# Moving the split of two weights from the recurrence's loop into its last tiles and the routing

## The chip, the cores and the metric

The program runs on one core of a Trainium2 chip, as one launch. The metric is the device time of one execution in microseconds (us), as the median of several runs. The kernel before takes 721.05 us (three runs, 720.83 to 721.4). For a change of this size a difference under about 0.2% (1.4 us) can't be told from none.

## The reference

Three stages follow one another, on 3072 tokens of width 384:

```python
# 1: gated linear recurrence; B, H, S, D = 4, 8, 768, 48
f = 1.0 / (1.0 + np.exp(-f_logit))
for t in range(S):
    state = f[:, :, t, :, None] * state + np.einsum('bhd,bhe->bhde', k[:, :, t], v[:, :, t])
    y[:, :, t] = np.einsum('bhd,bhde->bhe', q[:, :, t], state)
...
# 2: routing of each token to one of E = 8 experts by cosine, two layers (384 -> 1024 -> 384)
expert_idx = np.argmax(logits, axis=1)
h = np.maximum(x[mask] @ w1[e], 0.0)
out[mask] = gate_w[mask, None] * (h @ w2[e])
...
# 3: the gated block
a = x @ w1
b = x @ w2
h = a * b @ w3
return (h @ w_out).astype(np.float32)
```

Since nothing stands between the last two products, the kernel multiplies the weights first: `w34 = w3 @ w_out`, of 1024 x 384. It must be exact to nearly fp32, so every large product is made of three fp32r products: each operand is split into a high half (a rounded copy) and a low half (the whole less the high half), and hi\*hi + hi\*lo + lo\*hi is summed. This case is about where the high and low halves of `w3` and `w_out` are made.

## The kernel before, in words

**Recurrence.** 24 tiles of 128 time steps (NT = 24) are worked through in steps s = -3 to 24. Each engine has its own program, and `steps` gives all of them the same frame: steps -3 to 4 written out, steps 5 to 20 as a hardware loop of four steps a turn (m, u), steps 21 to 24 written out. In one step several tiles are in flight at different stages; `tile_of(s, lag)` says which tile a part of the step works on. The order in a step is fixed by hand on each engine, and the engines meet by semaphores alone:

- TensorE (PE): `scores` (L691) of tile s, `cumulate` (L682, L683) of s+2, `rows_and_logits` (L744) of s-1, `turn_qk` (L735) of s+1, then `state_products` (L703), `chunk_products` (L724) and `update_products` (L714) of s.
- ScalarE (ACT): `copy_yT` (L995) of s-1, the logarithms (L966 to L971) of s+3, the exponentials (L979, L981) of s+2, `copy_qT` (L986) of s+1, `square` (L998) of s-1. `rows_and_logits` of a tile waits for its `copy_yT`.
- VectorE (DVE): `carry` (L1212), `scale_k` (L1189), `mask` (L1205), `bound` (L1195), `take_rows` (L1224, L1226), `copy_kT` (L1200), `low_logs` (L1179). `scores` of the next tile waits for `copy_kT`.
- GpSimd (POOL): `decay` (L566), `clamp` (L552), `scale_q` (L558).

**The weights' halves in the loop.** SyncE loads one row block of `w3` (transposed, 128 x 1024) and one of `w_out` (128 x 384) every two steps. In each loop step ScalarE makes the high half of half a row block of `w3` (`high_w3`, L1010, 512 elements a partition) at the step's start and of half a block of `w_out` (`high_wo`, L1004, 192) at its end; GpSimd makes the low half of `w3` (`low_w3`, L575) and VectorE that of `w_out` (`low_wo`, L1174). In the profile numbers and endings are left out of names: `w_hi<-w_sb` at L1010 is `w3_hi`, `w_lo<-w_sb,w_hi` at L575 is `w3_lo`, and `w<-b_a` at L1081 is `w34_hi`.

**The end of the recurrence and the routing.** In step 23 VectorE looks for the smallest decay (`find_least`, L1270), and in step 24 TensorE turns that column (L793) and VectorE makes a flag of it. Then VectorE alone runs the routing: a chain of small instructions, each waiting for the one before (`link`), from L1357 to L1463. TensorE fills this time with the eight products of `w34` (`w34_product(f1)`, 24 matmuls each, L765 to L767) and takes part in the chain at four places, in this order: products 0 and 1, the ranks (L833, L834, wait for `rank_in`, set by the scan at L1365), products 2 and 3, the first list (L839, waits for `list_in`, set by L1390), products 4 and 5, the full list (L846), `turn(0)` (L857, waits for the first four gathers of GpSimd, L624, which wait for the `ids` made of the first list), products 6 and 7. Then come the experts' slots, from 182.47 us on, and the gated block.

**SBUF.** The halves of both weights lie over tiles of later stages; `w3_hi` overwrites `w3_sb` from one row block behind.

Of the kernel before, what the change touches and what calls it, by code (L numbers as in the profile page):

```python
# [27 lines left out]
P = 128  # L28
# [23 lines left out]
TURN_AT = 3  # L52
LISTS = 5
# [9 lines left out]
RING = 4  # L63
# [49 lines left out]
def build(nc, ctx, qkvf, emb, tau, sets1, sets2, w3_t, w_out, out):  # L113
# [22 lines left out]
    w3_lo = low_w3.enter_context(nc.sbuf_tensor("w3_lo", [P, KF, KF, P], F32R))  # L136
# [11 lines left out]
    early("rest_of_w3_lo", [P, KF * FF - KF * 2 * DM])  # L148
    x_all = early("x_all", [P, (RING + 1) * DM])
    wo_lo = early("wo_lo", [P, KF, DM], F32R)  # L150
    above = ExitStack()
    w3_hi = above.enter_context(nc.sbuf_tensor("w3_hi", [P, KF, FF], F32R))
    above.close()
    early("first_w3_hi", [P, FF])
    w3_sb = early("w3_sb", [P, KF, FF])
# [3 lines left out]
    early("first_wo_hi", [P, DM])  # L159
    wo_sb = early("wo_sb", [P, KF, DM])  # L160
    early("up_to_rows", [P, 1216])
# [141 lines left out]
    w3_hi_done, w3_lo_done, wo_lo_done = sem("w3_hi_done"), sem("w3_lo_done"), sem("wo_lo_done")  # L303
# [224 lines left out]
    def _(pool):  # L528
# [40 lines left out]
        def low_w3(m, u):  # L569

            rows = bass.ds(m * 2 - 2 + u // 2, 1)
            cols, places = slice(u % 2 * FF // 2, (u % 2 + 1) * FF // 2), slice(u % 2 * KF // 2, (u % 2 + 1) * KF // 2)
            by_place = lambda ap: ap.rearrange("p a (f n) -> p f (a n)", n=P)
            pool.wait_ge(w3_hi_done, m * 8 + (2 * u - 7))
            pool.tensor_tensor(w3_lo[:, places, rows, :].rearrange("p f a n -> p f (a n)"),  # L575
                               by_place(w3_sb[:, rows, cols]), by_place(w3_hi[:, rows, cols].bitcast(F32)),
                               ALU.subtract).then_inc(w3_lo_done, 1)
# [41 lines left out]
        pool.sem_inc(w3_lo_done, 2)  # L619
# [8 lines left out]

        pool.wait_ge(x_done, NT)
# [40 lines left out]
    def _(pe):  # L670
# [98 lines left out]
        def w34_product(f1, blocks=range(KF)):  # L769
            if 0 in blocks:  # L770
                pe.wait_ge(w3_lo_done, 2 * KF + 2)
                pe.wait_ge(wo_lo_done, 2 * KF + 2)
                if f1 >= 4:
                    pe.wait_ge(w34_hi_done, f1 - 3)
                    pe.wait_ge(w34_lo_done, f1 - 3)
            for f2 in blocks:
                cols = slice(f1 * P, (f1 + 1) * P)
                mm = three(W34_BANKS[f1 % 4][:, 0:DM], w3_hi[:, f2, cols], w3_lo[:, f1, f2, :], wo_hi[:, f2, :],
                           wo_lo[:, f2, :], f2 == 0, f2 == KF - 1)
            if KF - 1 in blocks:  # L780
                mm.then_inc(w34_done, 1)
# [181 lines left out]
    def _(act):  # L963
# [36 lines left out]
        def high_wo(m, u):  # L1000
            rows, half = bass.ds(m * 2 - 2 + u // 2, 1), slice(u % 2 * DM // 2, (u % 2 + 1) * DM // 2)
            act.wait_ge(w3_in[u // 2], m * 32)
            act.wait_ge(wo_lo_done, m * 4 + (u - 3))
            act.copy(wo_hi[:, rows, half], wo_sb[:, rows, half]).then_inc(w3_hi_done, 1)  # L1004

        def high_w3(m, u):
            rows, half = bass.ds(m * 2 - 2 + u // 2, 1), slice(u % 2 * FF // 2, (u % 2 + 1) * FF // 2)
            act.wait_ge(w3_in[u // 2], m * 32)
            act.wait_ge(w3_lo_done, m * 4 + (u - 3))
            act.copy(w3_hi[:, rows, half], w3_sb[:, rows, half]).then_inc(w3_hi_done, 1)  # L1010

        def step(s, r, part=None):
            if part:
                high_w3(*part)
# [17 lines left out]
            if part:  # L1032
                high_wo(*part)
# [6 lines left out]

        act.wait_ge(flag_done, 1)
# [121 lines left out]
    def _(dve):  # L1163
# [68 lines left out]
        def low_wo(m, u):  # L1232

            rows, half = bass.ds(m * 2 - 2 + u // 2, 1), slice(u % 2 * DM // 2, (u % 2 + 1) * DM // 2)
            dve.wait_ge(w3_hi_done, m * 8 + (2 * u - 6))
            low(wo_lo[:, rows, half], wo_sb[:, rows, half], wo_hi[:, rows, half]).then_inc(wo_lo_done, 1)

        def step(s, r, part=None):
# [74 lines left out]
        dve.sem_inc(wo_lo_done, 2)  # L1313
# [288 lines left out]
```

## Time and profile before

| | |
|---|---|
| median of 3 runs | 721.05 us |
| the profiled execution | 719.52 us, of which the span (first to last instruction) is 717.6 us |
| TensorE busy | 704.7 us, 98% of the span, granted clock 0.999 |
| VectorE, ScalarE, GpSimd busy | 347.1, 292.1, 193.8 us |
| loop steps 5 to 20 | 38.17 to 124.46 us (starts of `scores` of tiles 5 and 20) |
| steps 21 to 24 | 129.89 to 145.9 us |
| routing with the products of `w34` | 145.9 to 182.5 us |
| experts and gated block | 182.5 to 717.6 us |

The span is read as a row of stages in which TensorE is nearly always busy. What an edit is worth is then how much TensorE's idle time in its stage grows or shrinks. The instructions' times count from the start of the span.

### The profile page before, as it was taken

To read this page: it belongs to the slowest core of one execution; us is meant where nothing else is said; L and a number is where in the kernel's file an instruction comes from. 1 tells how busy PE (TensorE), PEld (TensorE's weight loads), DVE (VectorE), ACT (ScalarE), POOL (GpSimd) and SP (SyncE) were. 2 spreads that over 40 slices of the span, in tenths; PEclk is the share of its full clock that TensorE was granted. 3 is DMA by queue.
4 is the path that set the end of the run, shared out by engine and by line. 5 is a ranking of instruction groups with operands and counts; after the bars stand their busy time and mean duration, and the time that the engine had idled before them with its cause. 6 is when DMAs were issued, how large, how long until landed. Compare 5 with 4: busy or idle time off the path is not lost.

```text
span 717.6 us, 13946 instructions
## 1 busy us (share of the span) xinstructions
PE 704.7 (98%) x4863; PEld 642.2 (89%) x4863; DVE 347.1 (48%) x564; ACT 292.1 (41%) x559; POOL 193.8 (27%) x197
## 2 busy tenths in 40 slices
PE   7999999999999999999999999999999999999997
PEld 6988988899999999999999988988988989889887
DVE  6899999768764545546465431212212112112121
ACT  6777888525353435535445342123022022121220
POOL 4567777202322021100000003024033051150242
PEclk9999999999999999999999999999999999999999
DMA  7788886261745443434243330000000010000001
GB/s 221 225 242 227 235 237 176 67 186 58 222 146 161 132 132 99 139 114 133 89 119 118 112 90 1 1 22 23 0 33 11 0 44 0 11 33 0 22 22 44
DMA packets 73056, 70.79 MB, mean 99 GB/s; under 512 B 20520, under 2 KB 61480, under 8 KB 73024
## 3 DMA queue, kind: packets, MB, share of 16 engines
q1 hardware_dynamic: 69952, 60.95, 29.2%
q0 software_dynamic: 3072, 9.44, 4.1%
q8 instruction: 17, 0.28, 0.2%
q14 instruction: 15, 0.12, 0.1%
HBM read 60.88 MB, written 9.49 MB: 98 GB/s over the span
## 4 chain that ended last, share of the span: by engine, by line
PE 79%; DVE 2%; issue 1%; ACT 1%; POOL 1%; DMA 0%; POOLq 0%; ACTq 0%; DVEq 0%
PE b_a L765 10%; PE b_a L767 10%; PE b_a L766 10%; PE bank L767 9%; PE bank L765 9%; PE bank L766 9%; PE b_y L765 6%; PE b_y L766 6%; PE b_y L767 6%; PE bank L857 1%; PE bank L744 1%; PE b_y L724 1%; PE bank L735 1%; PE b_a L691 1%; DMA xs<-x_recurrence,ids 0%
## 5 line engine op out<-in xcount | busy, mean ns | idle before, releaser
L650 POOL TENSOR_TENSOR p_lo<-prod,p_hi 128x512 fp32r<-128x512 f32 x42 | 54.0, 1285 | 333.2 <-ACT p_hi L1149 333.2
L1146 ACT COPY a_sb<-b_a 128x512 f32<-128x512 f32 x48 | 28.3, 589 | 218.2 <-PE bank L767 218.2
L1551 DVE TENSOR_TENSOR prod<-bank,a_sb 128x512 f32<-128x512 f32 x48 | 33.2, 692 | 165.7 <-ACT a_sb L1146 165.7
L1507 DVE SCALAR_TENSOR_TENSOR h_lo<-b_a,h_hi 128x432 fp32r<-128x432 f32 x64 | 38.9, 607 | 96.0 <-ACT h_hi L1099 94.4
L1099 ACT ACTIVATE h_hi<-b_a 128x432 fp32r<-128x432 f32 x64 | 34.1, 532 | 124.2 <-PE b_a L767 116.3
L1174 DVE TENSOR_TENSOR w_lo<-w_raw,w_hi 128x768 fp32r<-128x768 f32 x72 | 67.9, 956 | 5.4 <-ACT w_hi L1062 1.2
L766 PE MATMUL b_a<-x_lo,w_hi 128*128 128x432 f32 x192 | 68.7, 358 | 0.0
L767 PE MATMUL b_a<-x_hi,w_lo 128*128 128x432 f32 x192 | 68.7, 358 | 0.0
L765 PE MATMUL b_a<-x_hi,w_hi 128*128 128x432 f32 x192 | 68.7, 358 | 0.0
L1062 ACT CAST w_hi<-w_raw 128x768 fp32r<-128x768 f32 x72 | 58.5, 834 | 0.0
L765 PE MATMUL b_a<-m_hi,w_hi 128*128 128x512 f32 x144 | 56.1, 390 | 0.7 <-DVE w_lo L1174 0.7
L767 PE MATMUL b_a<-m_hi,w_lo 128*128 128x512 f32 x144 | 56.1, 390 | 0.0
L766 PE MATMUL b_a<-m_lo,w_hi 128*128 128x512 f32 x144 | 56.1, 390 | 0.0
L765 PE MATMUL bank<-m_hi,w_hi 128*128 128x512 f32 x144 | 56.0, 389 | 0.0
L766 PE MATMUL bank<-m_lo,w_hi 128*128 128x512 f32 x144 | 56.0, 389 | 0.0
L767 PE MATMUL bank<-m_hi,w_lo 128*128 128x512 f32 x144 | 56.0, 389 | 0.0
L624 POOL DMA_INDIRECT xs<-x_recurrence,ids x24 | 26.0, 1084 | 110.9 <-PE bank L857 76.3
L765 PE MATMUL b_y<-h_hi,w_hi 128*128 128x432 f32 x128 | 46.9, 366 | 0.2
L766 PE MATMUL b_y<-h_lo,w_hi 128*128 128x432 f32 x128 | 45.8, 358 | 0.0
L767 PE MATMUL b_y<-h_hi,w_lo 128*128 128x432 f32 x128 | 45.8, 357 | 0.0
L766 PEld LDWEIGHTS b_a<-x_lo,w_hi 128*128 128x128 f32 x192 | 36.2, 188 | 1.4
L765 PEld LDWEIGHTS b_a<-x_hi,w_hi 128*128 128x128 f32 x192 | 36.1, 188 | 1.5
(247 smaller groups left out, 1630.2 us busy)
## 6 DMA issues: line engine op xcount, KB each, us to landing
w_raw<-sets SPq DMA_DIRECT2D x80, 192.0 KB, 3.8
w_raw<-sets SPq DMA_DIRECT2D x40, 384.0 KB, 4.6
ring_all<-qkvf SPq DMA_DIRECT2D x24, 384.0 KB, 3.9
ring_fc<-qkvf SPq DMA_DIRECT2D x24, 192.0 KB, 3.8
ring_all<-qkvf SPq DMA_DIRECT2D x24, 192.0 KB, 2.7
x_recurrence<-x_all SPq DMA_DIRECT2D x24, 192.0 KB, 3.5
w_sb<-w_t SPq DMA_DIRECT2D x8, 512.0 KB, 4.7
wo_sb<-w_out SPq DMA_DIRECT2D x8, 192.0 KB, 3.8
```

Source lines behind the costliest of these rows:

```text
L624: pool.indirect_dma_start(out=xs[:, w % BATCH, :], out_offset=None, in_=rec_dram.rearrange("b c p n -> (b c p) n"), in_offset=bass.Indirec ...
L650: pool.tensor_tensor(p_lo[:, f, :], prod[:, f % 2, :], p_hi[:, f, :].bitcast(F32), ALU.subtract).then_inc(pl_done, 1)
L691: mm = pe.matmul([b_a0, b_a1][g][:, j * P:(j + 1) * P], kT[g * HP:(g + 1) * HP, r % 2, j, :], qT[g * HP:(g + 1) * HP, r % 2, j, :], start= ...
L765: pe.matmul(acc, a_hi, b_hi, start=first, stop=False, skip_group_check=skip)
L766: pe.matmul(acc, a_hi, b_lo, start=False, stop=False, skip_group_check=skip)
L767: return pe.matmul(acc, a_lo, b_hi, start=False, stop=last, skip_group_check=skip)
L1062: act.copy(piece(w_hi, f), piece(w_raw, f)).then_inc(wh_done, 1)
L1099: act.activation(h_hi[:, f % 2, 0:SW], b_h[f % 2][:, 0:SW], ACT.Relu).then_inc(hh_done, 1)
L1146: act.copy(a_sb[:, f % 2, :], b_a[f % 2][:]).then_inc(as_done, 1)
L1174: return dve.tensor_tensor(out_, whole, high.bitcast(F32), ALU.subtract)
L1507: dve.scalar_tensor_tensor(out=h_lo[:, f % 2, 0:SW], in0=b_h[f % 2][:, 0:SW], scalar=0.0, in1=h_hi[:, f % 2, 0:SW].bitcast(F32), op0=ALU.m ...
L1551: dve.tensor_tensor(prod[:, f % 2, :], b_b[f % 2][:], a_sb[:, f % 2, :], ALU.mult).then_inc(pr_done, 1)
```

## The change

Nothing of the two weights is split in the loop any more; both are still loaded there. The work is done whole-block by whole-block:

- ScalarE makes the high half of `w_out` in two casts of 1536 elements a partition (steps 21 and 23) and that of `w3` in eight casts of 1024 (a column block f1 each): block 0 in step 21, 1 in step 22, 2 in step 23, 3 behind step 24, 4 and 5 behind the square root of the norms, 6 and 7 behind the first two copies of `w34`.
- VectorE makes the low half of `w_out` in two instructions of 1536 elements, at the end of steps 22 and 23.
- GpSimd makes the low half of `w3`, two instructions of 512 elements a block: block 0 in step 22, block 1 in step 23, blocks 2 to 7 behind the steps and ahead of the first gathers.
- TensorE waits for each product's own block, not for all of them.
- `low_logs` stands right behind `bound` on VectorE, ahead of `take_rows` and `copy_kT`.
- The raw, high and low blocks of `w3` share one tile and partly overwrite each other, three blocks apart; the SBUF layout follows.

```diff
-        def low_w3(m, u):
-            rows = bass.ds(m * 2 - 2 + u // 2, 1)
...
-            pool.wait_ge(w3_hi_done, m * 8 + (2 * u - 7))
-            pool.tensor_tensor(w3_lo[:, places, rows, :].rearrange("p f a n -> p f (a n)"),
...
+        def low_w3(f1):
+            pool.wait_ge(w3_hi_done, f1 + 1)
+            if f1 >= LOW_HEAD:
+                pool.wait_ge(w3_lo_done, f1 * 2)
+            for part in (slice(0, KF // 2), slice(KF // 2, KF)):
+                pool.tensor_tensor(w3_lo(f1)[:, part], w3_raw(f1)[:, part], w3_hi(f1)[:, part].bitcast(F32), ALU.subtract
+                                   ).then_inc(w3_lo_done, 1)
...
-            if part:
-                low_w3(*part)
+            if isinstance(s, int) and s == NT - 2:
+                low_w3(0)
             if isinstance(s, int) and s == NT - 1:
                 whole_constants()
                 counted_constants()
+                low_w3(1)
...
+        for f1 in range(2, KF):
+            low_w3(f1)
         pool.wait_ge(x_done, NT)
...
-                pe.wait_ge(w3_lo_done, 2 * KF + 2)
-                pe.wait_ge(wo_lo_done, 2 * KF + 2)
+                pe.wait_ge(w3_lo_done, f1 * 2 + 2)
+                pe.wait_ge(wo_lo_done, 1)
...
+            if KF - 1 in blocks:
+                pe.wait_ge(wo_lo_done, 2)
...
+        def high_wo(half):
+            rows = slice(half * KF // 2, (half + 1) * KF // 2)
+            act.wait_ge(w3_in[1], 16 * KF)
+            need(act, wo_lo_done, half)
+            act.copy(wo_hi[:, rows, :], wo_sb[:, rows, :]).then_inc(wo_hi_done, 1)
+
+        def high_w3(f1):
...
+            need(act, w3_lo_done, (f1 - HIGH_AHEAD + 1) * 2)
+            act.copy(w3_hi(f1), w3_raw(f1)).then_inc(w3_hi_done, 1)
 
         def step(s, r, part=None):
-            if part:
-                high_w3(*part)
             if (i := tile_of(s, -1)) is not None:
                 copy_yT(i)
...
-            if part:
-                high_wo(*part)
+            if isinstance(s, int) and s == NT - 3:
+                high_wo(0)
+                high_w3(0)
+            if isinstance(s, int) and s == NT - 2:
+                high_w3(1)
+            if isinstance(s, int) and s == NT - 1:
+                high_wo(1)
+                high_w3(2)
...
+        high_w3(3)
         act.wait_ge(flag_done, 1)
...
+        high_w3(4)
+        high_w3(5)
         for f1 in range(KF):
             act.wait_ge(w34_done, f1 + 1)
             act.copy(w34_hi[:, f1, :], W34_BANKS[f1 % 4][:, 0:DM]).then_inc(w34_hi_done, 1)
+            if f1 < 2:
+                high_w3(6 + f1)
...
+        def low_wo(half):
+            rows = slice(half * KF // 2, (half + 1) * KF // 2)
+            dve.wait_ge(wo_hi_done, half + 1)
+            low(wo_lo[:, rows, :], wo_sb[:, rows, :], wo_hi[:, rows, :]).then_inc(wo_lo_done, 1)
...
             if (i := tile_of(s, 2)) is not None:
                 bound(i)
+            if (i := tile_of(s, 3, 1)) is not None:
+                low_logs(i, r + 3)
...
-            if (i := tile_of(s, 3, 1)) is not None:
-                low_logs(i, r + 3)
-            if part:
-                low_wo(*part)
+            if isinstance(s, int) and s in (NT - 2, NT - 1):
+                low_wo(s - (NT - 2))
             if isinstance(s, int) and s == NT - 1:
                 find_least()
                 scale_experts()
```

The order of instructions at two places shows what moves. First ScalarE from the last `square` of the loop's tiles to the routing, before (`yT` is `copy_yT`, `x_all,nsq` is `square`):

```order
L998 ACTIVATE x_all,nsq<-x_all 128x384 [waits nsq_done,x_done]
L995 COPY yT<-b_y 128x512 [waits xl_at,y_done]
L986 COPY qT<-bank 128x512 [waits sp_done,tr_done]
L1027 ACT_TABLE_LOAD
L1027 ACTIVATE rt<-nsq 128x8 [waits rl_done]
L998 ACTIVATE x_all,nsq<-x_all 128x384 [waits nsq_done,x_done]
L995 COPY yT<-b_y 128x512 [waits xl_at,y_done]
L998 ACTIVATE x_all,nsq<-x_all 128x384 [waits nsq_done,x_done]
L995 COPY yT<-b_y 128x512 [waits xl_at,y_done]
```

And the same stretch of ScalarE in the changed kernel, whose line numbers are other (`w_high<-w_all` is a block of `w3`), up to the last copy of `yT`, which follows it:

```order
L1006 ACTIVATE x_all,nsq<-x_all 128x384 [waits nsq_done,x_done]
L1012 CAST wo_hi<-wo_sb 128x1536 [waits w3_in1]
L1018 CAST w_high<-w_all 128x8x128 [waits w3_in1,w3_in0]
L1003 COPY yT<-b_y 128x512 [waits xl_at,y_done]
L994 COPY qT<-bank 128x512 [waits sp_done,tr_done]
L1033 ACT_TABLE_LOAD
L1033 ACTIVATE rt<-nsq 128x8 [waits rl_done]
L1006 ACTIVATE x_all,nsq<-x_all 128x384 [waits nsq_done,x_done]
L1018 CAST w_high<-w_all 128x8x128 [waits w3_in1,w3_in0]
L1003 COPY yT<-b_y 128x512 [waits xl_at,y_done]
L1006 ACTIVATE x_all,nsq<-x_all 128x384 [waits nsq_done,x_done]
L1012 CAST wo_hi<-wo_sb 128x1536 [waits wo_lo_done,w3_in1]
```

Each of the three copies of `yT` now stands behind one or two casts. Second, GpSimd behind the steps, before (constants of the routing, then the first gather):

```order
L587 IOTA steps_k 128x56
L589 IOTA slot_no 1x152
L591 IOTA lane_no 128x1
L592 IOTA tile_no 128x24
L594 IOTA win_no 128x24
L595 IOTA row_no 128x128
L624 DMA xs<-x_recurrence,ids 128x384 [waits x_stored2,x_stored3,x_stored1,ids_done,x_stored0,x_done]
```

And in the changed kernel from the second instruction of block 2 on:

```order
L581 TENSOR_TENSOR w_lo_head<-w_all,w_high 128x512 [waits w3_hi_done]
L581 TENSOR_TENSOR w_lo_head<-w_all,w_high 128x512
L581 TENSOR_TENSOR w_lo_head<-w_all,w_high 128x512 [waits w3_hi_done]
L581 TENSOR_TENSOR w_lo_head<-w_all,w_high 128x512
L581 TENSOR_TENSOR w_lo_head<-w_all,w_high 128x512 [waits w3_hi_done]
L581 TENSOR_TENSOR w_lo_head<-w_all,w_high 128x512
L581 TENSOR_TENSOR w_high<-w_all,w_high 128x4x128 [waits w3_lo_done,w3_hi_done]
L581 TENSOR_TENSOR w_high<-w_all,w_high 128x4x128
L581 TENSOR_TENSOR w_high<-w_all,w_high 128x4x128 [waits w3_lo_done,w3_hi_done]
L581 TENSOR_TENSOR w_high<-w_all,w_high 128x4x128
L629 DMA xs<-x_recurrence,ids 128x384 [waits x_stored2,x_stored3,x_stored1,ids_done,x_stored0,x_done]
```

Ten of these instructions belong to blocks 3 to 7; GpSimd had nothing to do there before.

## Rows read from the trace of the kernel before

**Rows 1.** The page: busy time, share of the span and instructions of each engine.
```profile
PE 704.7 (98%) x4863; PEld 642.2 (89%) x4863; DVE 347.1 (48%) x564; ACT 292.1 (41%) x559; POOL 193.8 (27%) x197
```
**Rows 2.** The timeline of TensorE: start us, us, engine line op, out<-in.
```profile
16.25 1.16 PE L691 MATMUL b_a<-qT,kT 64*128 64x128 f32 x16
...
21.68 1.16 PE L691 MATMUL b_a<-qT,kT 64*128 64x128 f32 x16
...
101.83 1.16 PE L691 MATMUL b_a<-qT,kT 64*128 64x128 f32 x16
...
129.89 1.16 PE L691 MATMUL b_a<-qT,kT 64*128 64x128 f32 x16
```
**Rows 3.** The timeline of VectorE and GpSimd in two loop steps.
```profile
102.22 0.55 DVE L1189 TENSOR_TENSOR ks<-ring_all,en 128x384 f32<-128x384 f32 x1
102.29 1.62 POOL L575 TENSOR_TENSOR w_lo<-w_sb,w_hi  x1 [1.24 <-ACT w_hi L1010]
...
107.74 1.28 POOL L575 TENSOR_TENSOR w_lo<-w_sb,w_hi  x1 [1.20 <-ACT w_hi L1010]
107.85 1.59 DVE L1189 TENSOR_TENSOR ks<-ring_all,en 128x384 f32<-128x384 f32 x1
...
108.99 0.82 POOL L566 TENSOR_TENSOR state<-s_sum,e_all 128x192 f32<-128x192 f32 x1
```
**Rows 4.** The timeline of VectorE, one loop step.
```profile
99.89 0.69 DVE L1200 COPY kT<-bank 128x512 f32<-128x512 f32 x1
```
**Rows 5.** Groups by line and shape: count, busy us, mean ns, idle before.
```profile
L966 ACT ACTIVATE ef<-ring_fc 128x384 f32<-128x384 f32 x24 | 12.6, 525 | 2.3 <-DVE ring_fc L1296 2.3
L1010 ACT CAST w_hi<-w_sb x16 | 9.9, 617 | 0.0
```
**Rows 6.** The page's groups of instructions, same columns.
```profile
L1146 ACT COPY a_sb<-b_a 128x512 f32<-128x512 f32 x48 | 28.3, 589 | 218.2 <-PE bank L767 218.2
...
L1062 ACT CAST w_hi<-w_raw 128x768 fp32r<-128x768 f32 x72 | 58.5, 834 | 0.0
```
**Rows 7.** Instructions by their line: ns min/median/max, first and last start, forms.
```profile
L650 POOL TENSOR_TENSOR p_lo<-prod,p_hi x42: 1279/1285/1297, 427.0 to 698.2; 128x512 fp32r<-128x512 f32 x42
...
L1174 DVE TENSOR_TENSOR m_lo<-mT,m_hi x8: 1758/1759/1760, 336.8 to 651.2; 128x1536 fp32r<-128x1536 f32 x8
```
**Rows 8.** The timeline of ScalarE, last tiles.
```profile
134.56 0.19 ACT L998 ACTIVATION_READ_ACCUMULATOR x_all<-x_all 128x1 f32 x1
...
143.44 0.19 ACT L998 ACTIVATION_READ_ACCUMULATOR x_all<-x_all 128x1 f32 x1
...
147.27 0.19 ACT L998 ACTIVATION_READ_ACCUMULATOR x_all<-x_all 128x1 f32 x1
```
**Rows 9.** The timeline of TensorE, last tiles.
```profile
135.97 1.14 PE L744 MATMUL bank<-pick,yT 128*128 128x104 f32 x8
...
141.15 1.14 PE L744 MATMUL bank<-pick,yT 128*128 128x104 f32 x8 [0.48 <-ACT yT L995]
...
144.97 0.27 PE L793 MATMUL bank<-ident,least_e 128*1 128x128 f32 x1
```
**Rows 10.** The timeline of VectorE, routing.
```profile
147.64 0.34 DVE L1357 TENSOR_TENSOR scratch<-raw_logits,scale_e 128x192 f32<-128x192 f32 x1
...
149.97 0.56 DVE L1365 TENSOR_TENSOR_SCAN scratch<-restart,scratch 128x192 f32<-128x192 f32 x1
...
155.09 0.36 DVE L1377 TENSOR_TENSOR scratch<-scratch 128x192 f32<-128x192 f32 x1
...
157.51 3.35 DVE L1390 TENSOR_TENSOR ring_all<-row_no,rt 128x3072 bf16<-128x3072 f32 x1
```
**Rows 11.** The timeline of TensorE, routing.
```profile
153.26 0.28 PE L833 MATMUL bank<-scratch,before 128*128 128x8 f32 x2
...
162.03 0.33 PE L839 MATMUL bank<-scratch,ring_all 128*128 128x8 bf16 x7
...
172.78 0.44 PE L857 MATMUL bank<-ident,xs 128*128 128x128 f32 x2 [0.25 <-DMA xs<-x_recurrence,ids]
```

More of the change, by code:

```diff
@@ L52 @@
 TURN_AT = 3
+HIGH_AHEAD = 3
+LOW_HEAD = 6
 LISTS = 5
@@ L135, in build @@
     low_w3 = ExitStack()
-    w3_lo = low_w3.enter_context(nc.sbuf_tensor("w3_lo", [P, KF, KF, P], F32R))
+    w3_lo_head = low_w3.enter_context(nc.sbuf_tensor("w3_lo_head", [P, LOW_HEAD, KF, P], F32R))
     low_w3.close()
@@ L147, in build @@
     NXT = NTOK + SW
-    early("rest_of_w3_lo", [P, KF * FF - KF * 2 * DM])
-    x_all = early("x_all", [P, (RING + 1) * DM])
-    wo_lo = early("wo_lo", [P, KF, DM], F32R)
[L151 to L155, printed above, removed]
+    above = ExitStack()
+    w3_high = above.enter_context(nc.sbuf_tensor("w3_high", [P, KF, (HIGH_AHEAD + KF) * P], F32R))
+    above.close()
+    w3_all = early("w3_all", [P, KF, (HIGH_AHEAD + KF) * P])
+    w3_sb = w3_all[:, :, HIGH_AHEAD * P:]
+    block_of = lambda w, f1: w[:, :, f1 * P:(f1 + 1) * P]
+    w3_raw = lambda f1: block_of(w3_all, HIGH_AHEAD + f1)
+    w3_hi = lambda f1: block_of(w3_high, f1)
+    w3_lo = lambda f1: w3_lo_head[:, f1] if f1 < LOW_HEAD else block_of(w3_high, HIGH_AHEAD + f1 - 1)
+    wo_lo = early("wo_lo", [P, KF, DM], F32R)
     above = ExitStack()
@@ L158, in build @@
     above.close()
-    early("first_wo_hi", [P, DM])
+    early("first_wo_hi", [P, KF // 2, DM])
     wo_sb = early("wo_sb", [P, KF, DM])
-    early("up_to_rows", [P, 1216])
+    x_all = early("x_all", [P, (RING + 1) * DM])
+    early("up_to_rows", [P, 64])
     ring_all = early("ring_all", [P, RING * 3 * DM])
@@ L302, in build @@
     w3_in = [sem(f"w3_in{j}") for j in range(2)]
-    w3_hi_done, w3_lo_done, wo_lo_done = sem("w3_hi_done"), sem("w3_lo_done"), sem("wo_lo_done")
+    w3_hi_done, w3_lo_done, wo_hi_done, wo_lo_done = (sem(n) for n in (
+        "w3_hi_done", "w3_lo_done", "wo_hi_done", "wo_lo_done"))
     masks_done, pads_done = sem("masks_done"), sem("pads_done")
@@ L567, in decay @@
                                ).then_inc(s_done, 1)
-        def low_w3(m, u):
-            rows = bass.ds(m * 2 - 2 + u // 2, 1)
-            cols, places = slice(u % 2 * FF // 2, (u % 2 + 1) * FF // 2), slice(u % 2 * KF // 2, (u % 2 + 1) * KF // 2)
-            by_place = lambda ap: ap.rearrange("p a (f n) -> p f (a n)", n=P)
-            pool.wait_ge(w3_hi_done, m * 8 + (2 * u - 7))
-            pool.tensor_tensor(w3_lo[:, places, rows, :].rearrange("p f a n -> p f (a n)"),
-                               by_place(w3_sb[:, rows, cols]), by_place(w3_hi[:, rows, cols].bitcast(F32)),
-                               ALU.subtract).then_inc(w3_lo_done, 1)
+        def low_w3(f1):
[5 more added lines that the diff above has]
+                                   ).then_inc(w3_lo_done, 1)
         def whole_constants():
@@ L775, in w34_product @@
                     pe.wait_ge(w34_lo_done, f1 - 3)
+            if KF - 1 in blocks:
+                pe.wait_ge(wo_lo_done, 2)
             for f2 in blocks:
-                cols = slice(f1 * P, (f1 + 1) * P)
-                mm = three(W34_BANKS[f1 % 4][:, 0:DM], w3_hi[:, f2, cols], w3_lo[:, f1, f2, :], wo_hi[:, f2, :],
+                mm = three(W34_BANKS[f1 % 4][:, 0:DM], w3_hi(f1)[:, f2, :], w3_lo(f1)[:, f2, :], wo_hi[:, f2, :],
                            wo_lo[:, f2, :], f2 == 0, f2 == KF - 1)
@@ L998, in square @@
             return act.activation(sq_junk, rows, ACT.Square, accum_out=nsq[:, bass.ds(i, 1)])
[L1000 to L1010, printed above, removed]
+        def high_wo(half):
[4 more added lines that the diff above has]
+        def high_w3(f1):
+            act.wait_ge(w3_in[0], 16 * KF)
+            act.wait_ge(w3_in[1], 16 * KF)
+            need(act, w3_lo_done, (f1 - HIGH_AHEAD + 1) * 2)
+            act.copy(w3_hi(f1), w3_raw(f1)).then_inc(w3_hi_done, 1)
         def step(s, r, part=None):
-            if part:
-                high_w3(*part)
             if (i := tile_of(s, -1)) is not None:
@@ L1230, in take_logits @@
             return dve.tensor_copy(raw_logits[:].rearrange("p i e -> p (i e)")[:, run_of(i, E)], b_x[:, DM:DM + E])
[L1232 to L1236, printed above, removed]
+        def low_wo(half):
+            rows = slice(half * KF // 2, (half + 1) * KF // 2)
+            dve.wait_ge(wo_hi_done, half + 1)
+            low(wo_lo[:, rows, :], wo_sb[:, rows, :], wo_hi[:, rows, :]).then_inc(wo_lo_done, 1)
         def step(s, r, part=None):
```

2 lines of the change are left out of this document (removed).

## The prediction

> **What bounds the kernel now.** I read the page first: TensorE is busy 98% of the span [rows 1]. So the question of every edit is how much idle time of TensorE it takes away or makes. The list of who waited for whom shows little for TensorE, but matmul ends are modelled and can cover a wait, so I went by the period: the starts of `scores`. The first tiles come 5.43 us apart, 16.25 and 21.68; from 16.25 to 129.89 there are 20 steps in 113.64 us [rows 2]. Twenty steps at 5.43 us would be 108.6 us, so the loop loses 5.0 us. The reader is to see in the timeline where: in the steps that run long, `scale_k` on VectorE takes 1.59 us in place of 0.55, because it began 0.11 us after GpSimd's `low_w3` and ended 0.42 us after it; where VectorE was first, it takes 0.55 us and `low_w3` takes 1.62 in place of 1.28 us [rows 3]. Whoever starts first keeps the other out until it is nearly through (a blocked instruction saves about 0.14 us of its own start). `decay`, queued behind `low_w3`, then runs after `scale_k`, at 0.82 us: the two engines take turns [rows 3].
>
> **The loop.** It loses 16 `low_w3`, 32 casts of ScalarE and 16 `low_wo` of VectorE. TensorE's own instructions stay, so the period can't go under 5.43 us; the gain is between 0 and 5.0 us. I take 5.0, since the long steps come from the pair above and one half of it goes. What could come in its place: `low_logs` (0.55 us when free) now stands ahead of `copy_kT`, which ended at 100.58 [rows 4] while `scores` began at 101.83 [rows 2], so 1.25 us of slack become about 0.7. It is used up only if `low_logs` meets a whole `clamp` of GpSimd; without `low_w3` in front of it, I expect `decay` and `clamp` early in the step, beside `mask`.
>
> **The last tiles.** ScalarE's casts cost 617 ns for 512 elements [rows 5] and 834 ns for 768 [rows 6], so 0.85 ns an element: 1.49 us for 1536 and 1.05 us for 1024 (estimates from these rows). The flattest slope among ScalarE's rows, 525 ns for 384 [rows 5] and 589 ns for 512 [rows 6], would make it 1.10 and 0.85 us: the other end. A low half of 1536 on VectorE is 1.76 us [rows 7]. All clocks below are those of the trace before; the loop's 5.0 us come off at the end.
> - Step 21. `square` ends at 134.75 [rows 8]. Two casts, 2.54 us, and the copy of `yT`, 0.59 us [rows 6], end at 137.88. TensorE, which began L744 at 135.97 [rows 9], begins it at 137.9: 1.95 us lost.
> - Step 22. TensorE already waits for `yT` here, 0.48 us at 141.15 [rows 9], so the cast ahead of it counts in full: 1.05 us, together 3.0.
> - Step 23. `square` ends at 143.63 [rows 8] and 3.0, that is 146.63. The second cast of `w_out` ends at 148.1, VectorE's low half of it at 149.9, and behind that, in order, stands `find_least`, 0.24 us. TensorE turns the column at 150.2 in place of 144.97 [rows 9]: together 5.2 us. The copy of `yT`, ready at 149.8, hides under this.
>
> At the other end of the cast times the same three come to 1.4, 0.85 and 1.8, together 4.05 us.
>
> **The routing.** GpSimd has blocks 3 to 7 left, ten instructions of 1.28 us [rows 7]. Block 3 needs its high half, made behind the last `square`: 147.46 [rows 8] and 5.2 and 1.05 is 153.7. VectorE's chain begins at 147.64 [rows 10] and 5.2, so 152.8. From 153.7 on both want to read two tiles of SBUF, the pair of rows 3. VectorE's instructions are linked: each starts only when the one before has landed, and by then GpSimd's next has been waiting. So each two-input instruction of the chain stands behind one whole instruction of GpSimd, which comes every 1.35 us (1.28, less an overlap, and VectorE's share of 0.15 to 0.2). Reductions and one-input instructions fit in between.
> - Ranks. In the way of the scan are L1359, L1360, L1362 and the scan itself. GpSimd's first four end at 155.0, 156.3, 157.7 and 159.1, so the scan (0.56 us) ends at 159.5 in place of 150.53 [rows 10]. TensorE is there at 153.26 [rows 11] and 5.2, 158.46: 1.1 us lost.
> - List. L1368, L1372, L1373, L1374, L1376 and L1377 take the other six; L1377 starts at 167.05 in place of 155.09 [rows 10], 11.96 us later, and GpSimd is done. L1390 ended at 160.86 [rows 10], now at 172.8. TensorE is there at 162.03 [rows 11] and 6.3, 168.3: 4.6 us lost.
> - First gathers. They hang on the list through VectorE: from the end of L1390 to L857 it was 11.92 us [rows 10, 11], so 184.75. TensorE's own work brings it there at 172.53 (172.78 less its wait of 0.25 [rows 11]) and 10.9, 183.4: 1.3 us in place of 0.25, 1.05 lost. From here VectorE and TensorE are both about 12 us late, and nothing more opens between them. GpSimd is free for the gathers at 167.2, before the `ids` are made.
>
> Together 6.75 us. The ends: if VectorE were never held up, the scan would end at 155.7 and L1390 at about 165.9, both ahead of TensorE: 0. In the other direction, without the 0.14 us of overlap a turn, the ten turns cost up to 2.4 us more: 9.2 us.
>
> The Trainium skill, SBUF — State Buffer, section Who interferes with whom, says that a VectorE instruction with two SBUF inputs contends with a GpSimd instruction that reads SBUF, and that the loser blocks for the whole instruction. Rows 3 agree for 384 columns (1.59 against 0.55 us); the rule makes no exception for the 8 columns of L1372 to L1374, for which no row here has a neighbour on GpSimd. By the rule the sum is the one above; with those three excepted it is the second rival.
>
> **The sum.** -5.0 + 5.2 + 6.75 = +7.0 us. On the profiled execution's 719.52 us that is 726.5. This execution was 1.5 us under the median of 721.05, and the same step from the median gives 728.0, which I predict. From the experts on, 182.47 us, the programs are the same on all engines.
>
> **The rivals.**
> 1. VectorE is not held up in the routing, because the chain's instructions are short and slip in. For it: nothing in the trace shows a linked chain beside GpSimd. Against it: rows 3 twice. Then -5.0 + 5.2 = +0.2: 721.2 us.
> 2. Only wide instructions block. The three of 8 columns pass, but GpSimd's ten are the same, and L1376 to L1388 meet those left: L1390 would end near 171.0, 1.8 us less: 726.2 us.
> 3. Not slower: no blocking as in 1, and the casts at the flat slope. Then the last tiles lose 4.05 us against the loop's 5.0: 720.1 us. It decides from the point where the three delays come to under 5.0 us and the chain stays ahead of TensorE. Against it: L1010 and L1062, the same kind of cast from SBUF to SBUF, both lie on the steep slope.
> 4. The loop gives nothing back, because `low_logs` ahead of `copy_kT` makes `scores` late where `low_w3` did before: +12.0, 733 us. For it: half the slack goes. Against it: 0.7 us are left.
>
> **How the numbers follow.** Forecast 0.70 (its own range 725.5 to 731: casts at either end, 1.2 us; overlap, 2.3 us upward; 1 us of the loop), rival 1 0.11, rival 2 0.05, rival 3 0.07, rival 4 0.07. Below 721 lie rival 3 and a part of rival 1, above 732 most of rival 4 and a little of the forecast: the range is 721 to 732. Under 0.2% (1.4 us, about what can be told from no change) lie nearly all of rival 1 and half of rival 3; so slower 0.84, same 0.10, faster 0.06.
>
> **What would show it.** Right: `scores` 5.43 us apart in every step from 16.25 to the last tiles, and no `scale_k` over 1 us; TensorE idle before L744 of steps 22 and 23 by 1.5 to 2 us each, and about 2 us before it turns the column; in the routing, two-input instructions of VectorE of 1.2 to 1.5 us where they took 0.2 to 0.4, one for each of GpSimd's ten; TensorE idle about 1 us before the ranks and 4 to 5 us before the first list. Wrong: if those instructions keep their old durations (rival 1), if only the 8-wide ones do (rival 2), or if a `low_logs` over 1 us stands ahead of a late `copy_kT` (rival 4).

## The result, and the profile after

The kernel after takes 728.16 us (median of 6 runs, 726.82 to 729.44), the kernel before, timed beside it, 720.36 us (6 runs, 718.17 to 721.4): 1.0111 times as long, 95% interval 1.009 to 1.0132. Forecast were 728.0 us and a range of 721 to 732. The profiled executions, between which the terms below are measured, took 728.09 and 719.52 us: +8.6, of which 1.3 us lie at the start and are not of the change (below).

The page of the profile after, answering to [rows 1]: TensorE has 3.1 us more of busy time and one per cent less of a longer span.

```profile
PE 707.8 (97%) x4863; PEld 647.3 (89%) x4863; DVE 341.4 (47%) x550; ACT 290.0 (40%) x537; POOL 191.3 (26%) x197
```

The stretches of TensorE after, cut at the same events as in the forecast (start and end in us, their length, PE's busy time and instructions, its mean granted clock as a share of full speed, DMA share, GB/s):

```profile
17.53:126.37 108.84, 108.84 (x1642) 1.00 0.79 228
126.37:146.06 19.69, 14.83 (x197) 1.00 0.13 33
146.06:156.00 9.94, 9.94 (x52) 0.83 0.25 71
156.00:169.26 13.26, 8.93 (x53) 0.91 0.65 201
169.26:181.33 12.07, 12.07 (x97) 0.82 0.23 66
181.33:726.20 544.87, 539.96 (x2716) 1.00 0.22 68
```

Beside the starts of before the sum closes:

| stretch | before | after | difference | forecast |
|---|---|---|---|---|
| from the second tile's `scores` to those of step 21, 20 steps [rows 2] | 113.64 | 108.84 | -4.8 | -5.0 |
| from there to the turn of the column [rows 2, 9] | 15.08 | 19.69 | +4.6 | +5.2 |
| to the ranks [rows 9, 11] | 8.29 | 9.94 | +1.65 | +1.1 |
| to the first list [rows 11] | 8.77 | 13.26 | +4.5 | +4.6 |
| to the first gathered rows [rows 11] | 10.75 | 12.07 | +1.3 | +1.05 |
| from there to the end of the span | 544.82 | 544.87 | 0 | 0 |

That is +7.3 us. (The forecast's six terms come to +7.0; its 728.0 was that on top of 721.05, while the kernel before, timed beside, had 720.36. So the shift of the medians was 7.8 us, 0.8 more than forecast, and the total is nearer than the shift because the base was 0.7 us too high.) The other 1.3 us of the profiled execution lie ahead of the second tile's `scores`, which began at 17.53 instead of 16.25 [rows 2]: TensorE's granted clock rose from 0.5 to 1.0 (1.2 to 2.4 GHz) at 9.85 us instead of 5.71. That goes with the execution and not with the change: of two kernels below with the same program up to there, one (a_tail) had the first `scores` at 11.63 us (clock risen at 5.91), the other (a_fill) at 12.91 (risen at 10.17).

The starts of TensorE in the last tiles and the routing (start us, us, line, op; in brackets the idle time before it and who ended it):

```profile
134.07 1.14 PE L751 MATMUL bank<-pick,yT 128*128 128x104 f32 x8 [1.55 <-ACT yT L1003]
...
140.20 1.14 PE L751 MATMUL bank<-pick,yT 128*128 128x104 f32 x8 [1.43 <-ACT yT L1003]
...
146.06 0.27 PE L801 MATMUL bank<-ident,least_e 128*1 128x128 f32 x1 [1.88 <-DVE least_e L1286]
146.16 1.79 PE L751 MATMUL bank<-pick,yT 128*128 128x104 f32 x8
...
156.00 0.28 PE L841 MATMUL bank<-scratch,before 128*128 128x8 f32 x2
...
169.26 0.80 PE L847 MATMUL bank<-scratch,ring_all 128*128 128x8 bf16 x24 [4.33 <-DVE ring_all L1405]
...
181.33 0.94 PE L865 MATMUL bank<-ident,xs 128*128 128x128 f32 x7
```

The reader is to see two things. The three waits of the last tiles and the long one for the list are where the forecast put them. The waits for the ranks (L841) and for the gathers (L865) are not there, and yet their stretches are longer; what stands out in them is the clock, 0.83 and 0.82 in the stretches above. It fell to 0.5 from 146.38 to 149.79 us, behind the three waits, and from 166.86 to 173.69, inside and behind the wait for the list. In the kernel before it stood at 1.0 from 5.71 us to 715.69. L751, which takes 1.03 us at full clock, took 1.79 at 146.16.

ScalarE in step 21 shows why L751 was late: two casts between `square` and the copy of `yT`, at the steep slope of the forecast (1.49, 1.05 and 0.59 us estimated):

```profile
131.13 1.46 ACT L1012 CAST wo_hi<-wo_sb 128x1536 fp32r<-128x1536 f32 x1
132.49 1.04 ACT L1018 CAST w_high<-w_all 128x1024 fp32r<-128x1024 f32 x1
133.44 0.58 ACT L1003 COPY yT<-b_y 128x512 f32<-128x512 f32 x1
```

VectorE's chain in the routing, answering to [rows 10], beside GpSimd's low halves (here in runs of 6 and 4 instructions):

```profile
151.00 0.36 DVE L1374 TENSOR_TENSOR scratch<-scratch,rt 128x192 f32<-128x192 f32 x1
151.39 1.33 DVE L1375 TENSOR_TENSOR scratch<-scratch,rank_w 128x192 f32<-128x192 f32 x1
152.76 0.35 DVE L1376 TENSOR_REDUCE rt<-scratch 128x24 f32<-128x192 f32 x1
...
154.13 1.53 DVE L1380 TENSOR_TENSOR_SCAN scratch<-restart,scratch 128x192 f32<-128x192 f32 x1
...
156.99 0.17 DVE L1385 COPY rt<-bank 128x16 f32<-128x16 f32 x1
...
158.17 1.21 DVE L1388 TENSOR_TENSOR rt<-rt 128x8 f32<-128x8 f32 x1
159.41 0.17 DVE L1389 TENSOR_TENSOR rt<-rt 128x8 f32<-128x8 f32 x1
159.62 1.39 DVE L1391 TENSOR_TENSOR scratch<-scratch,rt 128x192 f32<-128x192 f32 x1
...
163.65 1.22 DVE L1398 TENSOR_SCALAR ring_fc<-ring_fc 128x24 f32<-128x24 f32 x1
164.90 0.18 DVE L1399 TENSOR_SCALAR ring_fc<-ring_fc 128x24 f32<-128x24 f32 x1
...
165.85 3.35 DVE L1405 TENSOR_TENSOR ring_all<-row_no,rt 128x3072 bf16<-128x3072 f32 x1
```
```profile
151.09 8.27 POOL L581 TENSOR_TENSOR w_lo_head<-w_all,w_high 128x512 fp32r<-128x512 f32 x6 [2.89 <-ACT w_high L1018]
159.50 5.33 POOL L581 TENSOR_TENSOR w_high<-w_all,w_high 128x512 fp32r<-128x512 f32 x4
```

Instructions of 192 and of 8 columns alike take 0.9 to 1.5 us in place of 0.2 to 0.6: they are held, one for each of GpSimd's. L1389, of 8 columns too, takes 0.17: GpSimd was idle when it began, from 159.35 to 159.50. The reduction (L1376) and the copy out of PSUM (L1385) slip in. One input is no protection: L1398 has one, of 24 columns in SBUF, and takes 1.22 us where L1399, behind GpSimd's last, takes 0.18.

### The profile page after: what moved, and what is told of

It reads as the page before. It is cut to its first block, busy times and chain, and to the rows that moved or that the text cites. A ratio compares the mean times of both kernels' runs of the same rounds, so it can differ in the third digit from the quotient of the medians.

```text
span 726.2 us, 13774 instructions
## 1 busy us (share of the span) xinstructions
PE 707.8 (97%) x4863; PEld 647.3 (89%) x4863; DVE 341.4 (47%) x550; ACT 290.0 (40%) x537; POOL 191.3 (26%) x197
## 4 chain that ended last, share of the span: by engine, by line
PE 91%; DVE 4%; issue 2%; ACT 2%; DMA 0%; DVEq 0%; POOLq 0%; POOL 0%; ACTq 0%
PE b_a L772 10%; PE b_a L773 10%; PE b_a L774 10%; PE bank L774 9%; PE bank L772 9%; PE bank L773 9%; PE b_y L772 6%; PE b_y L773 6%; PE b_y L774 6%; PE b_a L698 3%; PE b_y L731 3%; PE bank L751 3%; PE bank L742 3%; PE b_y L710 2%; PE b_y L721 1%
```

## The experiments

Each was timed beside the kernel before on its own chip; the medians of before were 719.6 to 719.9 us there. A profiled execution lies up to 1.7 us from its kernel's median, and the second tile's `scores` begin at 16.2 to 18.4 us in these traces, so terms are taken from stretches of the trace behind that point. From there to the gathered rows (L865) it is 163.80 us in the kernel after.

**The order in the last tiles (a_tail).** Each cast stands right behind a copy of `yT`: three of them in the step that they ended before, blocks 0 and 2 of `w3` one step on. The first low half of `w_out` is made in step 21 and no longer in 22, the second behind `find_least`:

```diff
         if (i := tile_of(s, -1)) is not None:
             copy_yT(i)
+        if isinstance(s, int) and s == NT - 3:
+            high_wo(0)
+        if isinstance(s, int) and s == NT - 2:
+            high_w3(0)
+            high_w3(1)
+        if isinstance(s, int) and s == NT - 1:
+            high_wo(1)
+        if isinstance(s, int) and s == NT:
+            high_w3(2)
...
+            if isinstance(s, int) and s == NT - 3:
+                low_wo(0)
...
             find_least()
+            low_wo(1)
             scale_experts()
```

> The kernel after, with the order of ScalarE's and VectorE's extra work in the last three steps changed and nothing left out: each cast of ScalarE now stands behind the copy of yT of the next step instead of ahead of it, and VectorE's second low half of w_out stands behind find_least. My theory (a cast costs TensorE time only because the copy of yT, or find_least, is queued behind it): TensorE's gaps ahead of L751 of steps 22 and 23 fall from 2.7 and 2.6 us to about 1.1 and 1.7, that ahead of L801 from 3.2 to 1.2, so the stretch from scores of step 21 on loses about 4.6 us; and the granted clock, which fell to 0.5 at 146.4 us behind these three gaps, stays at 1.0 there, another 1.7 us. Together 6.3 us: about 722. The wait for the ranks, which did not come, may then show by up to 1 us. Rival (what delays yT and find_least is not the queue but slower instructions beside GpSimd's low halves): the gaps stay and the time stays within 1 us of the kernel after, 727 to 729.

Measured: 721.83 us (10 runs, 720.59 to 722.95), 1.0034 of before (1.0021 to 1.0048): 6.3 us less than the kernel after, as expected; by the stretches of the traces it is 6.0. TensorE's waits in the same places:

```profile
136.49 1.14 PE L751 MATMUL bank<-pick,yT 128*128 128x104 f32 x8 [0.48 <-ACT yT L1003]
...
140.30 0.27 PE L801 MATMUL bank<-ident,least_e 128*1 128x128 f32 x1
...
149.75 0.39 PE L841 MATMUL bank<-scratch,before 128*128 128x8 f32 x2 [0.99 <-DVE scratch L1382]
...
162.25 0.76 PE L847 MATMUL bank<-scratch,ring_all 128*128 128x8 bf16 x24 [3.46 <-DVE ring_all L1407]
```

From the `scores` of step 21 to L801 it is 15.07 us, as before the change. The clock did not fall behind it. And the wait for the ranks is there, 0.99 us against the 1.1 forecast: in the kernel after, the slow clock had made TensorE so late that the ranks were ready first. The number came out, its parts did not: 4.6 us are from the last tiles, as expected, but only 0.5 from the stretch to the ranks, where the wait took the place of the slow clock, and 0.8 from the list, which the expectation did not have. (The clock fell once here, from 162.92 to 166.34 us, behind the wait for the list.)

**The list, without reading (a_memset).** GpSimd writes the low halves of blocks 2 to 7 without reading:

```diff
             for part in (slice(0, KF // 2), slice(KF // 2, KF)):
+                if f1 >= 2:
+                    pool.memset(w3_lo(f1)[:, part].bitcast(F32), 0.0).then_inc(w3_lo_done, 1)
+                    continue
```

> The kernel after, but GpSimd writes zeros over the low halves of blocks 2 to 7 of w3 (twelve memsets of 512 elements, about 0.5 us each) instead of working them out: left out are these low halves. It keeps GpSimd writing to SBUF beside VectorE's chain, but it reads nothing. Theory A (VectorE is kept out while GpSimd READS SBUF): no instruction of the chain is longer than in the kernel before (L1375 0.2 us, the scan 0.56), the list is there about 4.4 us sooner, the wait at L847 is gone or under 0.5 us, and the clock does not fall behind it: 6 us less, about 722. Theory B (any GpSimd instruction on SBUF keeps VectorE out for its length): the chain's two-input instructions still stand behind a memset each, 0.6 to 0.8 us instead of 0.2, up to twelve of them, and 2 us or more of the wait stay: 724 to 726.

Measured: 722.47 us (10 runs, 720.63 to 723.46), 1.0035 (1.0023 to 1.0047). Theory A holds. (The counterpart of L1375 took 0.36 us in the kernel before, L1360, not the 0.2 of the expectation.) Memsets and chain do run side by side, and the chain has its old durations:

```profile
150.29 0.99 POOL L582 MEMSET w_lo_head<- 128x512 f32 x2 [4.01 <-ACT w_high L1021]
```
```profile
150.24 0.36 DVE L1377 TENSOR_TENSOR scratch<-scratch,rt 128x192 f32<-128x192 f32 x1
150.63 0.36 DVE L1378 TENSOR_TENSOR scratch<-scratch,rank_w 128x192 f32<-128x192 f32 x1
```

From the ranks to the list it is 8.77 us, as before, and on to the first gathered rows 10.75, as before. The first fall of the clock, behind the last tiles, is still there, from 146.89 to 150.30 us (9.93 us to the ranks). A memset is also shorter, 0.5 us against 1.39, but a hold of its length would show on the two rows above.

**One input (a_one_input).** The same place, with `pool.tensor_scalar_mul(w3_lo(f1)[:, part], w3_raw(f1)[:, part], 0.0)` in place of the memset.

> The kernel after, but for blocks 2 to 7 GpSimd reads one tile instead of two: it multiplies the raw block by zero (twelve instructions of 512 elements) in place of working out the low half, which is left out. It stands between the kernel after (two tiles read: VectorE's chain late by 5.2 us between the ranks and the list, 728.2) and the run with memsets (nothing read: no delay, 722.5). Theory A (it is the second input on GpSimd that keeps VectorE out): the chain runs as with the memsets, L1375 takes 0.36 us, no wait for the list, 722 to 723. Theory B (any GpSimd instruction that reads SBUF keeps VectorE's two-input and SBUF-to-SBUF instructions out for its length): the chain is late again, in proportion to GpSimd's instruction, which by clamp (1.16 us for 384) would be 1.4 to 1.6 us, so 728 or up to 2 us more.

Measured: 724.21 us (5 runs, 722.65 to 724.35), 1.0063 (1.0043 to 1.0083). Neither theory has its number, A is the nearer. The list is in time (8.77 us from the ranks), though GpSimd is busy throughout, at 1.5 us an instruction:

```profile
149.31 9.07 POOL L582 TENSOR_SCALAR w_lo_head<-w_all 128x512 fp32r<-128x512 f32 x6 [1.43 <-ACT w_high L1021]
```

VectorE's instructions beside it are held up by 0.3 to 0.4 us and only some of them: L1378 takes 0.65 us, L1383 0.85, L1401 0.57, while L1377, L1380 and L1394 take their 0.36. In the other direction VectorE's write of the list (3.35 us) stretched one GpSimd instruction to 3.65. The chain is about 1 us later behind the list, and TensorE waits 1.35 us for the gathers. So GpSimd's two-input instructions hold long and its one-input ones do not. The two differ in the operation as well (a subtraction of two tiles, a product with a constant), so that it is the second input was not shown by itself; why a one-input instruction holds some for 0.3 us is open too.

**Shorter instructions (a_quarters).**

```diff
-            for part in (slice(0, KF // 2), slice(KF // 2, KF)):
+            for n in range(4):
+                part = slice(n * KF // 4, (n + 1) * KF // 4)
```

> The kernel after, with each low half of w3 in four GpSimd instructions of 256 elements instead of two of 512 (32 for 16; the sums are the same). My theory: a VectorE instruction that reads two tiles of SBUF stands behind one whole GpSimd instruction, so with instructions about half as long (some 0.7 us) each wait of the chain is about half: L1375, L1377, L1380, L1383, L1391, L1392 fall from 1.2 to 1.5 us to about 0.8, and the wait for the list (4.3 us at L847) falls by about 2 to 3 us, with the stretch at the lower clock behind it (1.7 us) perhaps gone: 723 to 726. Rival (what counts is how much GpSimd reads in all, in whatever pieces, as in a shared bandwidth): the chain ends as late as before and the wait stays 4 us or more: 727.5 to 729.

Measured: 727.83 us (4 runs, 726.57 to 728.99), 1.0106 (1.0082 to 1.013): the rival's number. The wait for the list is 3.67 us (4.33 after), a little under the rival's 4. The 0.7 us that the list gains are lost behind it: to the gathered rows it is 12.83 us in place of 12.07, at the lower clock up to 175.51 us. The holds did halve, but twice as many instructions were held:

```profile
151.18 0.77 DVE L1378 TENSOR_TENSOR scratch<-scratch,rank_w 128x192 f32<-128x192 f32 x1
...
163.35 0.71 DVE L1403 TENSOR_TENSOR scratch<-win_no,ring_fc 128x96 f32<-128x96 f32 x1
163.99 0.71 DVE L1404 SCALAR_TENSOR_TENSOR rt<-ring_fc,rt 128x24 f32<-128x24 f32 x1
```

From the copy behind the ranks to the start of the write of the list VectorE needs 8.86 us in the kernel after, 8.59 here and 3.65 with the memsets. My expectation was wrong: it halved the price of a turn and kept the number of turns. The chain alternates with GpSimd as long as GpSimd has work: behind the ranks it loses 5.2 us beside 7.8 us of GpSimd's work in the kernel after, and 4.9 us beside 8.6 us here.

**The clock (a_fill, a_fill_38).** Transposes of a constant keep TensorE at work while it waits for the list:

```diff
+        for _ in range(60):
+            pe.transpose(b_kT[:, 0:P], ident[:], ident[:])
```

> The kernel after, with 60 transposes of a constant on TensorE, results unused, between the fourth w34 product and the wait for the list, where TensorE stood still for 4.3 us. Theory (the products behind that wait took 10.3 us in place of 8.6 because the granted clock fell to 0.5 during the wait): the clock stays at 1.0 through the wait and the two products behind it, the list comes as late as before, and the time is 1.7 us less: about 726.4. Rival (the products are slow because their operands are still being written, or because ScalarE's copies out of PSUM hold them back): the products stay at 10.3 us and the time stays 728 to 728.5; if the transposes delay the products by running past the list, more.

Measured: 728.43 us (4 runs, 728.34 to 729.04), 1.0123 (1.0104 to 1.0143). The clock stayed at 1.0 from 150.12 us on, so also behind the list, the two products took 8.60 us (10.29 after), but the 60 transposes ran 2.2 us past the list. So once more with 38:

> The kernel after with 38 transposes ahead of the wait for the list in place of the 60 run before. Those took 112 ns each, 6.7 us in all, and ran 2.2 us past the arrival of the list, which ate what the two products behind it gained (8.60 us in place of 10.29). 38 take 4.25 us and end as the list arrives. By the theory that the lower granted clock behind the wait costs 1.7 us: the products take 8.6 us, nothing is delayed, and the time is 1.5 us or so less than the kernel after, 726.3 to 726.9. Rival: as with the 60, no gain, 728 or more.

Measured: 726.55 us (4 runs, 726.34 to 728.25), 1.009 (1.0067 to 1.0114). The 38 end 0.2 us ahead of the list, the products take 8.58 us, and then a wait opens:

```profile
165.02 4.31 PE L846 MATMUL bank<-ident 128*128 128x128 f32 x38
169.51 0.76 PE L849 MATMUL bank<-scratch,ring_all 128*128 128x8 bf16 x24 [0.18 <-DVE ring_all L1407]
...
181.28 1.53 PE L867 MATMUL bank<-ident,xs 128*128 128x128 f32 x12 [1.24 <-DMA xs<-x_recurrence,ids]
```

From the list to the gathered rows it is 11.77 us, 0.3 less than in the kernel after, not 1.7: the gathers were 1.24 us late all along, and the slow clock had covered them. The profiled execution, 728.25 us, is the slowest of the four; the other three lie at 726.3 to 726.6, as two of the six of the kernel after do (726.8). So the median can't tell 0.3 from 1.7 us here, and I go by the stretch.

**`low_logs` (a_logs_back).** In VectorE's step `low_logs` stands behind `copy_kT` again:

```diff
-            if (i := tile_of(s, 3, 1)) is not None:
-                low_logs(i, r + 3)
...
             if (i := tile_of(s, 1)) is not None:
                 copy_kT(i, r + 1)
+            if (i := tile_of(s, 3, 1)) is not None:
+                low_logs(i, r + 3)
```

> The kernel after, with low_logs back behind copy_kT in VectorE's step, where it was before the change. My theory (ahead of copy_kT it only uses slack): nothing moves by more than 0.3 us, scores stay 5.43 us apart, 727.5 to 729. Rival (the move itself costs, for example in the last tiles or at the ranks): 1 us or more less than the kernel after.

Measured: 728.61 us (4 runs, 726.96 to 729.39), 1.0115 (1.0089 to 1.0141): no difference from the kernel after. The move costs nothing and brings nothing.

**Both costs away (a_tail_memset).**

> Both edits at once: ScalarE's casts behind the copy of yT and VectorE's low half behind find_least, as in the run that gave 721.8, and GpSimd writing zeros over the low halves of blocks 2 to 7 instead of working them out, as in the run that gave 722.5; left out are these low halves. If the last tiles and VectorE's chain are the whole cost of the change, the time is that of the kernel before less the loop's 4.8 us, 715 to 716. If the two costs overlap, or there is a third, 717 or more.

Measured: 715.43 us (4 runs, 715.19 to 716.17), 0.9939 (0.9915 to 0.9962). 12.7 us less than the kernel after, where the two edits alone gave 6.3 and 5.7 (by the stretches 11.6, 6.0 and 5.8): all of the cost is in these two places, and what is left is the loop's gain. The clock stays at 1.0 from 5.27 to 711.83 us.

**The loop without the move (b_swap).** The kernel before, with `decay` at the end of GpSimd's step ahead of `low_w3`, one tile on:

```diff
             if (i := tile_of(s, 3, 3)) is not None:
                 before_clamp(i, r + 3)
-            if (i := tile_of(s, -2)) is not None and not (isinstance(i, int) and i >= NT - B):
-                decay(i, r + 2)
+                if part:
+                    pool.sem_inc(apart, 1)
...
                 scale_q(i, r + 1)
+            if (i := tile_of(s, -1)) is not None and not (isinstance(i, int) and i >= NT - B):
+                decay(i, r + 3)
             if part:
                 low_w3(*part)
```

(The semaphore `apart` is waited for by nobody.)

> The kernel before (all splitting still in the loop), with the order of GpSimd's loop step changed: decay, which waits for VectorE's s_sum, is moved from the front of the step to its end, straight ahead of low_w3, and becomes that of the next tile; so low_w3 no longer starts beside scale_k. Nothing is left out. My theory (the loop of the kernel before loses 5.0 us only because scale_k and low_w3 collide, not because there is 16 low_w3, 32 casts and 16 low_wo too much in it): scores come 5.43 us apart in every step, no scale_k over 1 us, the last tiles and the routing as before: 4.8 us less, about 715.3 beside a before of 720. Rival 1 (the loop is short of VectorE or GpSimd time whatever the order): low_w3 now collides with another instruction (mask, low_logs, copy of the logits) and the loss stays, 718 to 721. Rival 2: decay so late makes the state late for TensorE: slower, over 721.

Measured: 716.3 us (6 runs, 715.47 to 716.81), 0.9948 (0.993 to 0.9966): faster than both kernels, with nothing left out. In the loop the collision is gone; the groups of VectorE and GpSimd between 16 and 130 us (busy us, mean ns, idle before):

```profile
L1192 DVE TENSOR_TENSOR ks<-ring_all,en 128x384 f32<-128x384 f32 x21 | 11.6, 552 | 0.0
```
```profile
L576 POOL TENSOR_TENSOR w_lo<-w_sb,w_hi x16 | 20.5, 1281 | 0.2 <-issue 0.2
```

`scale_k` takes 552 ns on average (857 in the kernel before). The starts of `scores` are at most 5.5 us apart but for two: one of 5.63, that every kernel here has, and the second, of 6.83, where TensorE waits 1.21 us for `scale_q`; GpSimd's `clamp`, ahead of `scale_q`, had waited 4.96 us for its input, whose transfer SyncE issued behind others that took 7.93 us (6.43 in the trace of before). Two kernels without this edit, a_one_input and a_tail_memset, had 5.96 and 5.97 there. Whether any of it is the edit's stays open; these 1.4 us cover the 1 us by which the expectation (715.3) was missed.

## Why the prediction was right, point by point

- *The loop, -5.0.* Right: -4.8. `scores` come 5.43 us apart in every step from 17.53 to 126.37 but one of 5.63, and `scale_k` averages 557 ns:

```profile
L1196 DVE TENSOR_TENSOR lg_lo<-lg,lg_hi 128x384 fp32r<-128x384 f32 x21 | 11.8, 562 | 0.0
L1206 DVE TENSOR_TENSOR ks<-ring_all,en 128x384 f32<-128x384 f32 x21 | 11.7, 557 | 1.3 <-PE b_y L721 1.1 <-issue 0.2
```

  The cause was shown by b_swap, which keeps every instruction and changes only their order: it was the meeting of `scale_k` and `low_w3`, not the amount of work. Rival 4 (`low_logs` makes `scores` late) is out: `low_logs` averages 562 ns (1049 in the kernel before), and a_logs_back changes nothing.
- *The last tiles, +5.2.* The mechanism is shown by a_tail, the sum was 0.6 us high: 4.6. L751 of steps 22 and 23 and L801 came later by 1.6, a further 0.95 and a further 2.05 us, against 1.95, 1.05 and 2.2. The miss is in how the durations were added: three rows in a line were taken as 1.49 + 1.05 + 0.59 us, but each instruction starts about 0.1 us before the row of the last one ends (the cast at 132.49 begins inside the one that runs from 131.13 to 132.59), so three take 2.8 us from the end of `square`, not 3.1.
- *The ranks, +1.1.* The wait did not come, and 1.65 us came in its place from the clock. The step that failed is "TensorE is there at ... 158.46": it took 8.29 us for that stretch, as at full clock. The scan ended at 155.66 us; at full clock TensorE would have stood there at 154.35 (146.06 and 8.29), which is a wait of 1.3 us, and a_tail, where the clock stayed up, has one of 0.99. The scan ended 9.6 us behind the start of L801, forecast were 9.3, and that this is so near is in part luck. Three of GpSimd's instructions were in the way, not four, since L1374 began just ahead of the first. But the chain itself began 4.18 us behind L801, in place of 2.67 in the kernel before, which the forecast did not have: block 2 on GpSimd held two instructions of `scale_experts` ahead of the chain, which take 0.17 and 0.23 us in the kernel before and in a_memset:

```profile
145.07 3.13 POOL L581 TENSOR_TENSOR w_lo_head<-w_all,w_high 128x512 fp32r<-128x512 f32 x2 [2.82 <-ACT w_high L1018]
146.11 0.89 DVE L1294 TENSOR_SCALAR rt<-rt 128x8 f32<-128x8 f32 x1
147.27 0.96 DVE L1296 TENSOR_SCALAR scale_e<-rt,rtau 128x8 f32<-128x8 f32 x1
```

- *The list, +4.6.* Right: +4.5, a wait of 4.33 us. That GpSimd's reads cause it is shown by a_memset. Ten instructions were held, as counted, but not quite the ten named: L1374 and L1389 passed, and the one-input L1397 and L1398, which the forecast let slip in, were held in their place. A turn took 1.37 us (151.09 to 164.83 for ten), forecast were 1.35. Two figures of the working don't follow from it, and neither mattered: 172.8 less 168.3 is 4.5 us, not 4.6, and ten overlaps of 0.14 us are 1.4 us, not the 2.4 of the upper end.
- *The first gathers, +1.05.* The same failure as at the ranks: the wait is absent and 1.3 us are there. The clock was low up to 173.69 and cost 1.7 us on the products (10.29 against 8.58); with it up, the wait is 1.24 us (a_fill_38). Here the clock cost little by itself, 0.3 us, since it covered a wait that was due.
- *Rivals 1 to 3.* Blocking is there, so 1 and 3 are out; the 8-wide L1388 was held 1.0 us, so 2 is out.

That the six terms sum so near is partly luck: what the clock added beyond the two waits (0.55 us at the ranks, 0.25 at the gathers) stood against the 0.6 us too much in the last tiles. The forecast had no term for the clock at all.

The Trainium skill, TensorE: Matmul & The Clock Gate, section HAM oscillation — how this bites in real kernels, says that a kernel whose TensorE waits long between bursts pays for its lower clock behind the wait. The trace agrees at the list, where products behind a wait of 4.33 us took 10.29 us in place of 8.6; at 146.38 the clock fell behind three waits of at most 1.88 us each, with work between them, which a look for one long wait would not have found. The Trainium skill, SBUF — State Buffer, section Who interferes with whom, names a VectorE `tensor_scalar` among the instructions that can contend with GpSimd, when its operands meet conditions; I had counted them as free, and L1398 with its 1.22 us agrees with the page of the Trainium skill. Its rule that whoever comes second is held for the whole instruction fits GpSimd's two-input instructions here, but not its one-input ones: of 1.5 us they held VectorE for 0.4 at most.

## What to carry to other kernels

Where two engines keep each other out, look at which instructions start beside each other before moving work to another stage: one swap in GpSimd's order got back 3.3 of the 4.8 us that the move of 64 instructions got (the late second step, whose cause is open, is nearly all of the rest), and nothing had to be paid for it in the last tiles and the routing. Work put beside a linked chain cost it about two thirds of the time that the other engine read (5.2 of 7.8 us), and cutting that work into pieces of half the length hardly helped (4.9 us). Put work that nobody waits for behind the instruction that somebody does, and when a wait of TensorE is added, price what runs behind it at the lower clock too, but not on top of a wait that this would cover.

## What the runs showed of the hardware that was not expected

- A GpSimd instruction with two SBUF inputs (1.39 us) held up VectorE's two-input instructions and its `TENSOR_SCALAR` ones from SBUF to SBUF nearly to its end, of 8 columns as of 192 (0.17 to 1.21, 0.18 to 1.22, 0.36 to 1.33 us), but not reductions (0.35 us), a reciprocal (0.20 us at 147.03) nor copies out of PSUM (0.17 us). A memset held up none, a one-input instruction of 1.5 us only some, by 0.3 to 0.4 us.
- TensorE's granted clock fell to 1.2 GHz 2 us into a wait of 4.33 us, and stayed there for 6.8 us; behind three waits of 1.55, 1.43 and 1.88 us, with 4.7 and 4.0 us of work between them, it fell for 3.4 us, in all seven kernels that have them; behind the wait of 3.46 us in a_tail also for 3.4 us. After single waits of 0.48 us, of 0.99 us (the ranks in a_tail) and of 1.24 us (the gathers in a_fill_38) it did not.
